# First batch of attention worked on pair by pair, its upper rows normalised on their own, the second batch's keys and values loaded whole

## What is computed

```python
kv = np.einsum('bhsd,bhse->bhde', k, v)
out = np.einsum('bhsd,bhde->bhse', q, kv)
rms = np.sqrt(np.mean(out * out, axis=-1, keepdims=True) + 1e-06)
x = out / rms * g_norm                       # then laid out as 4608 x 512
x = (sigmoid(x @ w_gate) * (x @ w_val)) @ w_out          # 512 -> 1536 -> 512
h = x @ w_in                                              # 512 -> 2048
g = np.where(h <= -1, 0, np.where(h >= 1, h, (h + 1) ** 2 / 4))
return g @ w_out2                                         # 2048 -> 512
```

## Time and profile before

| | |
|---|---|
| median of 3 runs | 1670.04 us (1669.25 to 1670.78) |
| profiled execution | 1676.74 us, its span 1675.0 us |
| mean granted TensorE clock | 0.997 of full |
| PE busy | 1649.8 us, 98% of the span |
| PEld busy | 1620.5 us, 97% |
| DVE busy | 1218.2 us, 73% |
| ACT busy | 886.2 us, 53% |
| POOL busy | 195.3 us, 12% |
| DMA | 278.91 MB, mean 167 GB/s |

### The profile page before, as it was taken

The page is one execution under the profiler, slowest core; times in us unless marked ns, Lnnn a source line. Parts: engine busy times, 40 slices in busy tenths (PEclk is TensorE's granted clock), DMA queues, the critical chain, the costliest instruction groups (busy, mean ns, idle before and its releaser), DMA issues. The chain is left out here.

```text
span 1675.0 us, 31801 instructions
## 1 busy us (share of the span) xinstructions
PE 1649.8 (98%) x12471; PEld 1620.5 (97%) x12471; DVE 1218.2 (73%) x1733; ACT 886.2 (53%) x1612; POOL 195.3 (12%) x258
## 2 busy tenths in 40 slices
PE   8999999999999999999999999999999899999999
PEld 5899999999999999999999999999999899999999
DVE  5766777678777776867778877777777677676664
ACT  5666666655555554544445555555555444444442
POOL 2300001025223421100002500000001200000000
PEclk9999999999999999999999999999999999999999
DMA  7534444344568878645344433323538954444450
GB/s 267 176 125 145 130 146 146 108 132 132 191 208 293 287 242 279 240 157 155 116 140 154 160 117 142 125 113 132 172 136 282 310 176 138 141 128 126 127 133 32
DMA packets 229317, 278.91 MB, mean 167 GB/s; under 512 B 33072, under 2 KB 172848, under 8 KB 229168
## 3 DMA queue, kind: packets, MB, share of 16 engines
q1 hardware_dynamic: 217104, 233.35, 42.1%
q0 software_dynamic: 12064, 43.52, 8.2%
HBM read 156.76 MB, written 120.06 MB: 165 GB/s over the span
## 5 line engine op out<-in xcount | busy, mean ns | idle before, releaser
L1583 PE MATMUL x<-t_hi,v_lo 128*128 128x288 f32 x1664 | 496.3, 298 | 7.5 <-ACT c_kept L1041 2.9
L1584 PE MATMUL x<-t_lo,v_hi 128*128 128x288 f32 x1664 | 491.5, 295 | 0.0
L1585 PE MATMUL x<-t_hi,v_hi 128*128 128x288 f32 x1664 | 490.2, 295 | 0.0
L1583 PEld LDWEIGHTS x<-t_hi,v_lo 128*128 128x128 f32 x1664 | 312.4, 188 | 12.7 <-ACT c_kept L1041 3.8
L1585 PEld LDWEIGHTS x<-t_hi,v_hi 128*128 128x128 f32 x1664 | 313.8, 189 | 0.0
L1584 PEld LDWEIGHTS x<-t_lo,v_hi 128*128 128x128 f32 x1664 | 312.9, 188 | 0.1
L1583 PE MATMUL y<-t_hi,v_lo 128*128 128x288 f32 x832 | 248.2, 298 | 0.9 <-DVE gate L1106 0.8
L1584 PE MATMUL y<-t_lo,v_hi 128*128 128x288 f32 x832 | 245.7, 295 | 0.0
L1585 PE MATMUL y<-t_hi,v_hi 128*128 128x288 f32 x832 | 245.0, 295 | 0.0
L1583 PE MATMUL x<-v_hi,t_lo 128*128 128x256 f32 x576 | 163.1, 283 | 0.0
L1584 PE MATMUL x<-v_lo,t_hi 128*128 128x256 f32 x576 | 163.1, 283 | 0.0
(11 more groups left out here) (187 smaller groups left out, 3512.7 us busy)
## 6 DMA issues: line engine op xcount, KB each, us to landing
g_scratch<-c_tile SPq DMA_DIRECT2D x128, 288.0 KB, 2.4
gq<-g_scratch SPq DMA_DIRECT2D x64, 512.0 KB, 6.1
h_scratch<-gate SPq DMA_DIRECT2D x192, 144.0 KB, 2.0
hq<-h_scratch SPq DMA_DIRECT2D x32, 864.0 KB, 5.2
stage<-w_in POOLq DMA_DIRECT2D x68, 256.0 KB, 3.9
kv_ring<-kv_in SPq DMA_DIRECT2D x30, 512.0 KB, 4.4
fold_hi<-v_hi SPq DMA_DIRECT2D x14, 896.0 KB, 6.3
fold_lo<-v_lo SPq DMA_DIRECT2D x14, 896.0 KB, 7.5
```

What stands on the lines that cost most here:

```text
L1583: nc.tensor.matmul(dst, s_lo, m_hi, start=start, stop=False, skip_group_check=True)
L1584: nc.tensor.matmul(dst, s_hi, m_lo, start=False, stop=False, skip_group_check=True)
L1585: return nc.tensor.matmul(dst, s_hi, m_hi, start=False, stop=stop, skip_group_check=True)
```

## The change

- SP loads K and V of batch 0 by pairs: for each pair c, the 128 columns of K and of V for rows 0 to 511 (two copies of 256 KB, runs of 512 B), then this pair's queries. The last 64 rows of all pairs come in one copy behind pair 0. They lie in places of their own (`first_kv`, `first_q`, where v_hi of tasks 2 to 5 comes later).
- Batch 1's five chunks go to a place of their own (`second_kv`) and are issued without a wait, and so are its first two queries.
- TensorE works `first_pair(c)` and `first_heads(0, c)` for pairs 0 and 1, their means, then pairs 2 and 3 and their heads. `first_bank` gives each pair a bank.
- Root, reciprocal and split of the inverse are done twice for batch 0: for pairs 0 and 1, and for all four (`root(0)`, `root(1)`; later batches count one higher). The spreads of pairs 0 and 1 come before step 0, those of 2 and 3 behind product 1 of step 0.
- All chunks of batch 1 come in step 0: two behind product 1, three behind product 5.
- The sums of task 1 move from VectorE to GpSimd, the low half of task 0 from VectorE (one operation) to GpSimd (seven, `split_first`).
- The 13 padding passes behind the first chunk go. The 10 at the start stay.
- ScalarE's order ahead of step 0 is new: square and scale pair by pair.

```diff
         @block.sync
-            def load_first_kv(i):
-                rows = min(P, S - i * P)
-                sp.dma_start(first_chunk(i)[0:rows, :], kv_in[0, i * P:i * P + rows, :]).then_inc(first_kv_loaded[i], 16)
+            def load_first_kv(c):
+                for side in range(2):
+                    at = slice(DM * side + P * c, DM * side + P * (c + 1))
+                    sp.dma_start(first_kv[:, 0:KVC - 1, at],
+                                 kv_in[0, 0:N, at].rearrange("(i p) d -> p i d", p=P)).then_inc(first_kv_loaded[c], 16)
...
             def load_kv(n, i):
-                j = KVC * (n - 1) + i
-                sp.wait_ge(kv_used, j + 1 if j < 2 else j + 4)
...
+                if n == 1:
+                    sp.dma_start(second_kv[0:rows, i, :], src).then_inc(second_kv_loaded[i], 16)
...
-            for i in range(KVC):
-                load_first_kv(i)
             for c in range(K):
+                load_first_kv(c)
+                if c == 0:
+                    sp.dma_start(first_kv[0:REST, KVC - 1, :], kv_in[0, N:S, :]).then_inc(first_rest_loaded, 16)
                 load_query(first_query(c), 0, c, first_q_loaded[c])
             sp.dma_start(g_col[:], g_in).then_inc(g_loaded, 16)
-            load_kv(1, 0)
-            load_kv(1, 1)
+            for i in range(KVC):
+                load_kv(1, i)
             load_q(1, 0)
             load_q(1, 1)
-            load_kv(1, 2)
-            load_kv(1, 3)
             for i in range(2):
                 load_query(q_second[:, i, :], 1, 2 + i, second_q_loaded[i])
-            load_kv(1, 4)
...
         @block.gpsimd
+            def split_first():
+                pool.wait_ge(v_hi_done, 1)
+                for x in range(SEVEN):
+                    done = nc.gpsimd.tensor_tensor(v_lo[:, x, :], stage[:, 0, x, :], v_hi[:, x, :].bitcast(f32), ALU.subtract)
+                done.then_inc(v_ready, 1)
...
-            pool.wait_ge(first_kv_loaded[3], 16)
+            pool.wait_ge(first_kv_loaded[1], 32)
             load_task(0)
-            pool.wait_ge(first_q_loaded[1], 32)
+            pool.wait_ge(first_kv_loaded[3], 32)
             load_task(1)
...
-                if FOLD2_TASK <= task < C_TASK:
+                if task == 0:
+                    split_first()
+                elif FOLD2_TASK <= task < C_TASK:
                     sum_right(task)
-                elif task >= 2:
+                else:
                     sum_left(task)
...
         @block.scalar
             def split_weights(task):
                 act.wait_ge(stage_summed, 4 * (task + 1))
+                if task == 2:
+                    act.wait_ge(kv_used, KVC)
+                    act.wait_ge(head_done, K)
...
-            def root(n):
-                act.wait_ge(ms_done, K * (n + 1))
-                reach(act, inv_ready, n)
+            def root(r):
+                act.wait_ge(ms_done, K * r if r else 2)
+                reach(act, inv_ready, r)
...
-            square_heads(0, 0)
-            scale_heads(0, 0)
-            for c in range(1, K):
+            for c in range(2):
                 square_heads(0, c)
+                scale_heads(0, c)
+            root(0)
             split_weights(0)
-            scale_heads(0, 1)
-            root(0)
+            split_inverse(0)
+            square_heads(0, 2)
+            square_heads(0, 3)
+            split_item(0, 0)
+            root(1)
             scale_heads(0, 2)
             scale_heads(0, 3)
-            split_inverse(0)
+            split_item(0, 1)
+            split_inverse(1)
             split_weights(1)
-            split_item(0, 0)
-            split_item(0, 1)
             nc.scalar.activation(table_col[:], eps_col[:], ACT.Sigmoid)
...
         @block.vector
+            def copy_first(c):
+                dve.wait_ge(first_kv_done, c + 1)
+                for j in range(P // D):
+                    rows = slice(j * D, (j + 1) * D)
+                    nc.vector.tensor_copy(kv_raw[rows, c, rows], first_bank(c)[rows, rows]).then_inc(kv_copied, 1)
...
-            copy_kv(0)
+            copy_first(0)
+            copy_first(1)
             sum_weights(0)
-            sum_weights(1)
-            split_weights(0)
+            copy_first(2)
             invert(0)
+            copy_first(3)
             split_inverse(0)
             normalize_part(0, 0, 0)
...
             split_item(0, 0)
             sum_item(0, 1)
+            invert(1)
+            split_item(0, 1)
+            split_inverse(1)
             normalize_part(0, 2, 0)
             normalize_part(0, 3, 0)
-            split_item(0, 1)
             normalize_part(0, 2, 1)
...
         @block.tensor
+            def first_pair(c):
+                pe.wait_ge(first_kv_loaded[c], 32)
+                if c == 2:
+                    pe.wait_ge(kv_copied, 2)
+                elif c == 3:
+                    pe.wait_ge(o_ready, 1)
+                for i in range(KVC):
+                    rows = min(P, S - i * P)
+                    if c == 0 and i == KVC - 1:
+                        pe.wait_ge(first_rest_loaded, 16)
+                    chunk = first_kv[:, i, :]
+                    last = nc.tensor.matmul(first_bank(c)[:, 0:P], chunk[0:rows, c * P:(c + 1) * P],
+                                            chunk[0:rows, DM + c * P:DM + (c + 1) * P],
+                                            start=i == 0, stop=i == KVC - 1, skip_group_check=True)
+                last.then_inc(first_kv_done, 1)
...
                     if (s, number) == (0, 1):
-                        kv_chunk(1, 3)
+                        kv_chunk(1, 0)
+                        kv_chunk(1, 1)
+
+                        pe.wait_ge(inv_ready, 2)
+                        pe.wait_ge(o_ready, K)
+                        pe.wait_ge(x_ready, 4)
+                        for c in (2, 3):
+                            for h in range(2):
+                                spread_part(0, c, h)
                     elif (s, number) == (0, 5):
-                        kv_chunk(1, 4)
+                        for i in range(2, KVC):
+                            kv_chunk(1, i)
...
             keep_warm(WARM_START)
-            for i in range(KVC):
-                kv_chunk(0, i)
-            keep_warm(WARM_COPY)
-            for c in range(K):
+            for c in range(2):
+                first_pair(c)
                 first_heads(0, c)
-            for c in range(K):
+            for c in range(2):
                 first_mean(0, c)
-            kv_chunk(1, 0)
-            kv_chunk(1, 1)
-            keep_warm(WARM_ROOT)
-            for c in range(K):
-                spread(0, c)
-                if c == 2:
-                    keep_warm(WARM_FIRST)
-            kv_chunk(1, 2)
+            for c in (2, 3):
+                first_pair(c)
+            for c in (2, 3):
+                first_heads(0, c)
+
+            pe.wait_ge(inv_ready, 1)
+            pe.wait_ge(spread_const, 1)
+            pe.wait_ge(o_ready, 2)
+            spread_part(0, 0, 0)
+            spread_part(0, 0, 1)
+            pe.wait_ge(kv_copied, 2 * K)
+            spread_part(0, 1, 0)
+            first_mean(0, 2)
+            pe.wait_ge(x_ready, 1)
+            spread_part(0, 1, 1)
+            first_mean(0, 3)
```

More of the change, by code:

```diff
@@ L908, in _ @@
                 if s == 2 and b + 1 < B:
-                    root(b + 1)
+                    root(b + 2)
                 if s == 4 and more:
@@ L1369, in _ @@
                 if s == 2 and b + 1 < B:
-                    invert(b + 1)
+                    invert(b + 2)
                 if s == 3 and b + 1 < B:
```

99 lines of the change are left out of this document (55 added, 44 removed).

## The result

The changed kernel takes 1678.71 us (median of six runs, 1675.92 to 1680.28) against 1671.39 us for the kernel before beside it: 1.0039 of its time, with a 95% interval of 1.0025 to 1.0052, or 6.5 us slower (0.0039 x 1671; the two medians themselves are 7.3 us apart, and a ratio over all runs need not be that of two medians). The forecast was no change, 1670.0 us in a range of 1667.0 to 1673.2. It was wrong, on the slow side.

The account below looks back on a forecast made before the run. TensorE is bound by when its continuous stream starts, gated by v_lo of task 1: 26.0 + 12.7 + 0.6 = 39.3 us, against 39.31 before. So no change: 1670.0 us, range 1667.0 to 1673.2.

Parts of the forecast that it names:

- Where the time would be decided: Nothing after 60 us changes; the change acts only through when TensorE gets its continuous stream.
- the gate: Product 1 of step 1, which waits for VectorE's v_lo of weight task 1; v_lo forecast to end at 39.3 us, as before.
- T_g: Landing of g, behind batch 0's loads, where scale(0) starts: 14.2 + 0.8 = 15.0 us, bounds 13.0 and 17.
- a scale(0) at 10 us: Sign at the start on ScalarE that would show the forecast wrong; scale(0) was expected near 15 us.
- From T_g to the first product: Batch 0's scaling, mean, root, reciprocal, spreads, item 0's split: 2.8 + 8.2 us to 26.0, first product about 26.1.
- Rival (b): TensorE idles four microseconds from about 12.6 us, its clock falls, mean and pair 2 slow: +2, 1672.0 us; chance 0.22.
- (d): Short runs or weights beside them delay batch 0's loads: T_g at 17 or 18, 1672.5 us; chance 0.08.
- First product to gate: Stretch to v_lo of task 1 with a second normalisation: 12.7 us plus 0.6 for GpSimd encounters.
- T: End of the split of item 0, just ahead of the first product: 26.0 us forecast, 28.54 before.
- (a): At the start g does not hold ScalarE; task 0's stage is next, reciprocal from 17.2, gate 37.0, 1667.7 us; chance 0.20.
- (c): GpSimd's eleven operations ahead of the gate become the bound, at 1.1 us each: gate 43.3, 1674.0 us; chance 0.08.
- What nobody paid for: Batch 1's loads, the stores of x and task 2's load were forecast to cost nothing at the start.

Follow-up runs that it names:

- 14 + 6 passes: The changed kernel with 14 padding passes between the means of pairs 0 and 1 and 6 in step 0, g last: 1.0016 of before.
- the two padded kernels with the same loads: The changed kernel, g last, with 14 or 20 padding passes between the first two means and 6 in step 0: 1.0016 of before each.
- g first: The changed kernel with the load of g issued ahead of everything, nothing else changed: 1.0006 of before.
- three kernels at full clock: The changed kernel with 20 and 6, or 14 and 6, padding passes (1.0016 each), or with g issued first and 6 and 6 (1.0009 of before).
- the shortened reciprocal: The changed kernel with g issued first and 6 and 6 padding passes, second reciprocal of batch 0 over 8 of 288 columns: 0.9993 of before.
- the other order: The changed kernel with g issued first, 3, 4 and 3 padding passes, second reciprocal and inverse split ahead of item 1, v_lo earlier: 1.0000 of before.
- with padding: The changed kernel with g issued first, 6 padding passes between the first two means and 6 in step 0: 1.0009 of before.
- 1 KB runs: The changed kernel with K and V of batch 0 loaded by two pairs, four copies of 512 KB, g still last: 1.0021 of before.

## Why the prediction was wrong, step by step

**Where the time would be decided: right.** The work after 60 us did not change, and the gate's delay of 5.7 us is the loss. Over the kernels of the table the timed difference follows the gate at about one microsecond to one, with a scatter of up to 2.4 us.

**The sum, term by term.** The forecast put the gate's product at 39.35 us; it came at 45.07. The 5.7 us are these (full-clock durations from the run with 14 + 6 passes). That they come close to the loss against before is because the forecast put the gate where before had it:

| term | forecast | measured | difference |
|---|---|---|---|
| T_g, start of scale(0) | 15.0 | 17.00 | +2.0 |
| scale(0) to first product, full clock | 11.1 | 12.08 | +1.0 |
| the clock in that part | 0 | 1.29 | +1.3 |
| first product to gate, full clock | 13.25 | 13.27 | 0.0 |
| the clock in that part | 0 | 1.43 | +1.4 |

**T_g: mechanism right, size off.** ScalarE stood for g exactly as argued; "a scale(0) at 10 us" did not happen. But the rate of 342 GB/s came from one microsecond of four loads that ran alone, and the price of 0.8 us for the short runs became 2.8 (17.0 against 14.2). With the queries between them, from 2 to 8 us, such loads got 276, and 258 and 285 in the two padded kernels with the same loads. The upper bound, 17 us, was stated and was the value, but its reason, weights mixed in, doesn't hold for these six microseconds: they are issued from 9.68 us on. In those two kernels g landed at 16.03 and 15.69 us, so 0.7 to 2.0 us is what this term was short by, and the 2.0 of this trace is its far end.

**From T_g to the first product: short by 1.0.** The mean came at T_g + 2.76 (forecast 2.8). Behind it, pair 2 took 1.57 us and not 1.26, for its passes cost 0.157 each on their own; the copy of pair 3 (0.47 for both halves) stands ahead of the inverse's low half on VectorE; and t_lo took 1.02 us beside a GpSimd sum where 0.76 was used. In the changed kernel itself that last one took 0.75 and the next operation, t_sum, 1.28: one encounter of 0.3 to 0.5 us, about as priced.

**The clock: named as a rival, with the wrong chance, place and size.** Rival (b) had TensorE idle for four microseconds, the fall, and the slow mean and pair 2. All of it occurred: 4.65 us of idle time, 1.65 and 2.66 us. It was given 0.22 and +2. The first fall cost less than its 2.3 us: 1.3, since the mean took 1.65 us against 1.17 and pair 2 took 2.66 against 1.57. The prediction's sentence that the 13 passes "had only filled waits" put their removal at nothing in the forecast; the kernel before without them shows the clock at 0.50 from 26 to 32 us, with no wait over 1.57 us behind the first chunk. And its reading that before has no hole over 1.00 us after 5 us is wrong: TensorE waits 5.03 us near 1314 us, with the clock at 0.50 behind it, in the very trace that it was read from. What the rival missed is the second fall, after TensorE's wait of 1.32 us for the second half's inverse, which stretched the 24 passes to 4.66 us, 1.4 us ahead of the gate. Step 0's last sum, and v_lo of task 1 behind it on VectorE, follow those passes: VectorE waited 0.91 us for the product. The prediction had no low clock in that part and let VectorE's waits take back some of the first fall; they took nothing back.

**Both together.** The decisive error is in how the cases were added. (b) and (d) stood as separate cases of 0.22 and 0.08, at 1672.0 and 1672.5 us, and a second term beside one of them only as a part of 0.13. But neither excludes the other: g's late landing lengthens TensorE's wait, the padding that might have filled it is gone, and the clock falls on a chain that is already late. In the runs they add: the clock's 2.7 us are there with g last and 2.6 with g first (41.79 against 39.15). With (d)'s +2 to 3 and (b)'s full 2.3, and nothing taken back, the forecast's own terms would have said 1674 to 1675; with what was measured for the clock (2.7) and for the way to the first product (1.0) it is 1676 to 1677.

**First product to gate: right, term by term.** 12.7 + 0.6 was forecast and three kernels at full clock gave 13.27 to 13.28. It is 3.3 us longer than before's 9.97, and cancels what two halves win at the first product. Some 0.8 us of this are no cost of the change: before's first product starts 0.85 us after T, behind a chunk of batch 1, and the new one 0.06. From T to the end of v_lo it is 10.77 us before and 13.27 with 14 + 6 passes, 2.5 more, and VectorE's rows there show the terms of the sum: the reciprocal 1.93, the second low half 0.45, the wait for its spread 0.56, one encounter of 0.53 (t_sum 1.28 instead of 0.75), and the wait of 0.89 for product 2 gone; together 2.6. This is VectorE's share and not a price for each: the shortened reciprocal moved nothing, and the other order only 0.5 us. In the changed kernel itself the wait for product 2 is back, 0.91 us, through the second fall of the clock.

**Rivals (a) and (c).** (a) did not occur. Where it was made to (g first), the stage was next, as it said, but with sums to 18.3 and a reciprocal at 18.9 us instead of 17.2, since the weights landed at 16.8 and not at 15; the gate with padding was at 39.15 and not 37.0 us. (c) did not occur: 0.73 us for each subtraction, and GpSimd's sums not on the path. The Trainium skill, SBUF — State Buffer, Who interferes with whom, has a VectorE operation outside its 2-port modes in GpSimd's way only when it has two SBUF inputs, and the seven subtractions, at 0.73 each while VectorE mostly ran the reciprocal, agree.

**What nobody paid for: right.** The loads of batch 1, the stores of x and task 2's load made no wait at the gate; the 0.72 us in front of it is the same wait for v_lo as before's 0.71.

## What to carry to other kernels

When a change moves work ahead of a wait, look up what the wait is for and where it stands on its queue: half a kilobyte at the end of 2 MB held the whole start here, and issuing it first won back 3.3 us at the gate (2.2 with the clock full), more than any of the reordering. A rival that lengthens a wait and a rival that lets the clock fall in that wait aren't alternatives; add them. And passes of padding are part of an order of work: whoever removes them has to point to what keeps TensorE busy in the same waits.

## What the hardware showed that I had not expected

- Loads by pairs in 512 B runs, with the queries between them, moved 276 GB/s between 2 and 8 us (258 and 285 in two kernels with the same loads), where whole rows of 4 KB moved 374 to 375, with a mean DMA share of 0.97 to 1.01; 1 KB runs moved 283. Alone, late in the kernel, short runs had shown 342. The Trainium skill, DMA: Bandwidth & Descriptors, Specifications, gives 512 B as the smallest transfer that reaches line rate; by that rule short and long runs would have been alike, and these rows disagree, though the number and order of the copies changed with the runs.
- A load of 0.5 KB behind such copies landed 5.8 us after its issue at 11.19 us (5.2 after 10.44 and 10.77 in the two padded kernels with the same loads), and with 1 KB runs 7.4 us after its issue at 7.88: an earlier issue moved the landing by half of what it moved the issue, or less. Issued first, at 0.75 us, it took 2.0.
- The clock fell to its 1.2 GHz level not only after idle times of 3.93 and 4.65 us, but also after waits of 0.70 and 1.25 us between short groups (g first), and again in the changed kernel after one of 1.32 us; in "g first" the same wait, of 1.05 us, was not followed by a fall. Nor were the waits of 2.72 us in the changed kernel and 3.00 us with 14 + 6 passes near 1314 us, where 3.99, 4.14 and 5.03 us in three other traces were. What decides between them these runs don't show; the length of the last wait alone doesn't. At the low level ten passes of 128 columns took 2.66 to 2.80 us against 1.57, and 24 passes of which most fell into it 4.66 against 3.03.
